# Attention tails in their units' rows, step 0's products between the attention units, and x's operands made by VectorE and ScalarE at the chunk ends

## What is computed

```
kv  = einsum('bhsd,bhse->bhde', k, v)             # 4 batches, 8 heads, 576 tokens, head size 64
out = einsum('bhsd,bhde->bhse', q, kv)
x   = out / sqrt(mean(out^2 over e) + 1e-6) * g_norm     # then [2304 tokens, 512]
h = x @ w_in1;  g = h * sigmoid(1.702 h);          x = g @ w_out1     # 512 -> 2048 -> 512
h = x @ w_in2;  g = max(h,0) + log1p(exp(-|h|));   out = g @ w_out2
```

## Time and profile before

| | |
|---|---|
| median of 3 runs | 854.32 us (853.38 to 855.62) |
| the profiled execution | 852.89 us, span 850.9 us |
| PE busy | 811.4 us, 95% of the span |
| DVE busy | 589.1 us, 69% |
| ACT busy | 417.4 us, 49% |
| POOL busy | 262.9 us, 31% |
| DMA | 139.26 MB, mean 164 GB/s |
| granted PE clock, 40 slices | 0.9 or more in all |

### The profile page before, as it was taken

How to read it: one execution, slowest core, us unless ns; L and a number is a source line. 1 busy time by engine, 2 the same in 40 slices (tenths; PEclk the granted TensorE clock), 3 DMA queues, 4 the chain that set the end, 5 groups by cost and what they waited for, 6 DMA issues and landing times.

```text
span 850.9 us, 12328 instructions
## 1 busy us (share of the span) xinstructions
PE 811.4 (95%) x4584; PEld 731.5 (86%) x4584; DVE 589.1 (69%) x1012; ACT 417.4 (49%) x800; POOL 262.9 (31%) x292
## 2 busy tenths in 40 slices
PE   6888999999999999999999998997999998999998
PEld 5788999988999988999987887886889887899896
DVE  3677567596656586666587777678776778776774
ACT  3663333233122133233257775665666665866765
POOL 4997787122124102345234423052100031000000
PEclk9999999999999999999999999999999999999999
DMA  9955646332843722854833544223252422262312
GB/s 309 339 211 177 239 152 267 154 112 87 284 173 122 275 87 88 301 221 155 309 126 112 212 168 166 86 96 122 104 186 87 172 89 87 97 237 87 108 67 74
DMA packets 25674, 139.26 MB, mean 164 GB/s; under 512 B 2448, under 2 KB 8208, under 8 KB 18448
## 3 DMA queue, kind: packets, MB, share of 16 engines
q1 hardware_dynamic: 25040, 138.16, 44.9%
q10 hardware_dynamic: 576, 0.33, 0.1%
HBM read 104.40 MB, written 34.08 MB: 163 GB/s over the span
## 4 chain that ended last, share of the span: by engine, by line
PE 74%; DVE 13%; ACT 5%; DMA 5%; issue 3%; ACTq 0%; DVEq 0%
PE ps L628 35%; PE ps L683 15%; PE ps L691 14%; PE ps L688 8%; DMA kv_in_sb<-k_v 4%; DVE gs_f L971 2%; DVE gs_f L1012 2%; DVE ex L1009 2%; DVE gs_f L1016 2%; DVE gs L1020 2%; DVE xs L946 2%; ACT gs L816 1%; ACT ex L792 1%; ACT fix L794 1%; ACT ex L790 1%
## 5 line engine op out<-in xcount | busy, mean ns | idle before, releaser
L628 PE MATMUL ps<-xs,w_in 128*128 128x384 f32 x2016 | 412.9, 340 | 23.6 <-DVE gs_f L971 16.5
L628 PEld LDWEIGHTS ps<-xs,w_in 128*128 128x128 f32 x2016 | 355.9, 188 | 56.6 <-issue 16.2
L683 PE MATMUL ps<-w_out,gs 128*128 128x512 f32 x864 | 228.0, 396 | 0.6 <-DVE gs L1020 0.4
L971 DVE TENSOR_TENSOR gs_f<-ps,gs_f 128x384 f32<-128x384 f32 x240 | 132.9, 555 | 137.2 <-PE ps L628 136.3
L683 PEld LDWEIGHTS ps<-w_out,gs 128*128 128x128 f32 x864 | 160.8, 189 | 25.8 <-issue 2.2
L691 PE MATMUL ps<-gs,w_out 128*128 128x512 f32 x576 | 148.2, 392 | 0.0
L691 PEld LDWEIGHTS ps<-gs,w_out 128*128 128x128 f32 x576 | 105.6, 188 | 16.4
L452 POOL TENSOR_TENSOR w_in<-w_in_f,w_in 128x256 fp32r<-128x256 f32 x112 | 93.5, 872 | 71.3 <-ACT w_in L821 71.0
L784 ACT ACTIVATE lg<-gs_f 128x384 f32<-128x384 f32 x72 | 37.8, 525 | 133.9 <-DVE gs_f L971 133.9
L816 ACT CAST gs<-gs_f 128x384 fp32r<-128x384 f32 x96 | 49.0, 510 | 94.0 <-DVE gs_f L1016 93.1
L1020 DVE TENSOR_TENSOR gs<-gs_f,gs 128x384 fp32r<-128x384 f32 x96 | 59.3, 617 | 41.3 <-ACT gs L816 38.2
(11 more groups left out here) (66 smaller groups left out, 571.1 us busy)
## 6 DMA issues: line engine op xcount, KB each, us to landing
w_in<-w_kept SPq DMA_DIRECT2D x40, 1792.0 KB, 7.4
w_kept<-w_in SPq DMA_DIRECT2D x16, 1792.0 KB, 10.4
kv_in_sb<-k_v SPq DMA_DIRECT2D x16, 512.0 KB, 10.8
w_in_f<-w_in SPq DMA_DIRECT2D x16, 512.0 KB, 4.1
w_out_f<-w_out SPq DMA_DIRECT2D x16, 512.0 KB, 8.1
q_sb<-q_t SPq DMA_DIRECT2D x16, 288.0 KB, 11.1
out<-xy SPq DMA_DIRECT2D x18, 256.0 KB, 7.8
tail_sb<-k_v SPq DMA_DIRECT2D x3, 256.0 KB, 12.5
```

The source lines that it names most:

```text
L628: mm = nc.tensor.matmul(ps[:, bank, 0:HALF], w[:, wp, W_OF[k], cols], xs[:, k, xp, t], start=(new and t == 0 and (wp, xp) == (HI, HI)), st ...
L683: mm = nc.tensor.matmul(ps[:, acc_bank(1, j), 0:DM], g[:, j * P:(j + 1) * P], w, start=new, stop=done)
L971: nc.vector.tensor_tensor(to, bank, other, ALU.add).then_inc(added, 1)
```

## The change

Four parts.

1. **k and v.** The host lays out k and v anew: per partition the four tiles of an even unit, then a tile whose rows 0 to 63 are its tail of k and the rest zero, a tile with both units' tails of v, then the odd unit's four tiles and a tile with its tail of k in rows 64 to 127. Each unit is one transfer (5120 or 4608 bytes a partition, before 4096 and the tails apart). `kv_in_sb` has 3 slots of two units, q 6 slots instead of 8. `tail_sb`, its memset and its four transfers are gone. ACT waits for the gain before its first `gain`, no longer before its second copy. The raw `w_in` of pair 2 and `w_out` of pair 0 are loaded after all units.
2. **Step 0.** P1 after unit 10, P2 (now second) after unit 12, P6 after unit 14; ACT copies C11 out of PSUM (`keep_c11`), so that the bank is free. U2 and U3 stand before unit 15's scaling. POOL makes x's slots before weight pair 2. DVE makes x's raw sums two by two behind units 9 and 10, before one by one behind units 9 to 12.
3. **Chunk ends.** POOL makes nothing of x. DVE makes the four sums of the late ends in the third and second step from the end (`ahead`) and all low parts, ACT all roundings. At the ends of layer 1 the same instructions stand in other places.
4. **`w_out` of layer 2** for pairs 6 and 7 is swapped in steps 26 and 28, not 24 and 25.

```
-    Q_SLOTS = 8
+    KV_SLOTS = 3
+    Q_SLOTS = 6
-        X_EARLY = (B11, B21, T2, T3, T4, T1, B22)
+        X_EARLY = (B11, B21, B22, T2, T3, T4, T1)
-        SWAP_FROM = PHASE1 - STEPS + 2
+        SWAP_AT = (18, 19, 20, 21, 22, 23, 26, 28)
 # SP
-                if u >= UNIT_SLOTS:
-                    sp.wait_ge(kv_done, u - UNIT_SLOTS + 1)
+                if u >= 2 * KV_SLOTS:
+                    sp.wait_ge(kv_done, (u // 2 - KV_SLOTS) * 2 + 2)
+                sp.dma_start(kv_in_sb[:, u // 2 % KV_SLOTS, kv_piece(u)], k_v[u // 2, :, kv_piece(u)]
+                             ).then_inc(kv_in[u % (2 * KV_SLOTS)], 16)
-            W_AT = {1: 0, 4: 1, 8: 2}
+            W_AT = {1: 0, 4: 1}
+            load_w_out(0, 0)
+            load_raw(2)
             keep(0)
 # PE, after unit u
-                if u == UNITS - 3:
+                if u == P1_UNIT:
                     product(0, P1)
+                if u == P2_UNIT:
+                    product(0, P2)
                 if u == UNITS - 2:
                     product(0, P6)
 # ACT, in a step; "late" is the end of steps 31 and 39
+                if ends_late:
+                    round_x(ci + 1, B11)
+                if begins_late:
+                    round_x(ci, T4)
+                    round_x(ci, T1)
                 if m > PHASE1:
                     round_g(m - 1, C12)
...
+                if ends_late:
+                    round_x(ci + 1, T2)
+                    round_x(ci + 1, B21)
+                if begins_late:
+                    round_x(ci, B22)
                 if m >= PHASE1:
                     round_g(m, C11)
...
+                if ends_late:
+                    round_x(ci + 1, T3)
                 hidden(m, C21)
 # DVE, in a step
+                ahead = X_LATE_FROM <= ci + 1 < 2 * CHUNKS and p in (STEPS - 3, STEPS - 2)
+                if begins and ci < X_LATE_FROM:
+                    low_x(ci, T3)
                 if m > 0:
                     add(m, U2)
                 if m > PHASE1:
                     low_g(m - 1, C12)
                 if begins:
                     low_x(ci, T4)
+                if ends or ends_late:
+                    low_x(ci + 1, B11)
+                if ahead:
+                    raw_x(ci + 1, T3 if p == STEPS - 3 else T4)
                 if phase:
                     add(m, U3)
                     softplus(m, C11)
...
+                if ends_late:
+                    low_x(ci + 1, T2)
+                if begins:
+                    low_x(ci, T1)
                 if phase:
                     low_g(m, C11)
                 add(m, C21_ADD)
...
+                if ends_late:
+                    low_x(ci + 1, B21)
                 if begins:
                     low_x(ci, B22)
+                if ahead:
+                    raw_x(ci + 1, T2 if p == STEPS - 3 else T1)
                 add(m, C22_ADD)
...
                 if ends:
-                    low_x(ci + 1, T3)
+                    low_x(ci + 1, B21)
+                    low_x(ci + 1, T2)
```

More of the change, by code:

```diff
@@ L57, in build @@
     UNITS, _, S = q_t.shape
+    KV_ROW = k_v.shape[2]
     T, DM = out.shape
@@ L188, in turn_bank, with kv_piece, kv_tile @@
             return TURN_ODD if u % 2 else TURN_EVEN
+        def kv_piece(u):
+            even = (2 * MAIN + 2) * P
+            return slice(even, KV_ROW) if u % 2 else slice(0, even)
+        def kv_tile(u, t):
+            slot = u // 2 % KV_SLOTS
+            first = kv_piece(u).start + 2 * t * P
+            k = kv_in_sb[:, slot, first:first + P]
+            if t == MAIN:
+                first = 2 * MAIN * P
+            return k, kv_in_sb[:, slot, first + P:first + 2 * P]
         def q_tokens(u, slot):
@@ L215, in g_high, with products_done @@
             return gs[:, m % 2, f, HI, half * HALF:(half + 1) * HALF]
+        P1_UNIT, P2_UNIT = 10, 12
+        def products_done(m, k):
+            place = {P2: P6, P6: P2}.get(k, k) if m == 0 else k
+            return PRODUCTS * m + place + 1
         def split_buffer(d):
@@ L600, in product @@
                         pe.wait_ge(x_split_early, X_EARLY.index(k) + 1)
-                    elif m // STEPS >= X_LATE_FROM and k in (B11, B21):
-                        pe.wait_ge(x_split_late, 2 * (2 * (m // STEPS - X_LATE_FROM) + (B11, B21).index(k) + 1))
                     else:
@@ L977, in _ @@
                     dve.wait_ge(x_made, 2 * PAIRS)
-                if 0 <= u - 2 * PAIRS - 1 < 4:
-                    raw_x(0, X_RAW_ORDER[u - 2 * PAIRS - 1])
-            add(0, U2)
+                    raw_x(0, T3)
+                    raw_x(0, T2)
+                if u == 2 * PAIRS + 2:
+                    raw_x(0, T4)
+                    raw_x(0, T1)
             def hidden_of(m, tile):
-                return ps[:, BANK_A, 0:HALF] if tile == C11 else hid(m, tile)
+                return ps[:, BANK_A, 0:HALF] if tile == C11 and m > 0 else hid(m, tile)
             def gate(m, tile):
@@ L1026, in _ @@
                 ends, begins = p == STEPS - 1 and m < ALL - 1, p == 0 and ci > 0
-                own_sums = ends and ci + 1 < X_LATE_FROM
+                ends_late = ends and ci + 1 >= X_LATE_FROM
+                ends = ends and not ends_late
+                ahead = X_LATE_FROM <= ci + 1 < 2 * CHUNKS and p in (STEPS - 3, STEPS - 2)
                 if m > PHASE1:
@@ L1040, in _ @@
                     softplus(m, C11)
-                elif m == 0:
-                    add(m, U3)
-                    gate_product(m, C11)
-                else:
+                elif m > 0:
                     gate_product(m, C11)
@@ L1065, in _ @@
                     low_x(ci, B22)
+                if ahead:
+                    raw_x(ci + 1, T2 if p == STEPS - 3 else T1)
+                add(m, C22_ADD)
+                if m == 0:
+                    gate_split(m, C11)
                 if phase:
```

202 lines of the change are left out of this document (84 added, 118 removed).

## The result

| | before | after |
|---|---|---|
| median of the runs | 854.41 us (853.38 to 855.62, 4 runs) | 830.03 us (828.63 to 830.67, 4 runs) |
| profiled execution | 852.89 us, span 850.9 | 830.67 us, span 828.9 |
| step 1's P1 starts at | 68.44 us | 62.98 us |

The ratio is 0.9712, with a 95% interval of 0.9694 to 0.973: the change is 2.9% faster. 830 us lies inside the range, 6 us above the forecast of 824.

What follows compares the result with a forecast made beforehand. PE's own pace was taken as the bound, with 31.0 us of waits around chunk ends and in steps 25 to 29, besides attention waits. Terms 7.0 + 5.9 + 17.6 = 30.5 us gave 824 us, range 816 to 836.

Steps and rivals of the forecast that it cites:

- Late ends: Steps 25 to 29, 31 to 33, 39 and 40: without POOL's work on x, 17.6 us saved; bounds 9 and 20.
- Ends of layer 1: Steps 7, 8, 15, 16, 23 and 24: reordered DVE work removes waits, 5.9 us saved; bounds 3 and 9.
- The new wait of P6 behind T2's low part: Ends of layer 1: P6 comes 1.1 us late in step 8, 0.4 in step 16, some 1.3 in step 24.
- Attention: Attention and step 0: step 1's P1 comes at 61.4 us and a C22 wait goes, 7.0 us saved; bounds 3 and 9.
- The start: I take 1.6 us: Start of the attention: the 1.74 us wait for tails goes, less a bigger kv of unit 0; 1.6 us saved.
- Rival 1: Attention: transfers keep holding it, at 300 GB/s step 1 starts at 65 us; 827.5 us, chance 0.13.
- Pair 2, moved last, is ready at 67 for step 2 at 77: Attention's end: POOL's work on weight pair 2, moved last, is ready at 67 us, ahead of step 2 at 77.
- Rival 2: Chunk ends: new waits take half the gain, 12 us instead of 23.5; 835.5 us, chance 0.13.
- Rivals 3 to 5: All waits go, 816.3 us, chance 0.08; slower through DVE's and ACT's queues, 867, 0.02; nothing that counts, 854, 0.01.

Runs made afterwards that it cites:

- b_late: Kernel before with only the two chunk ends inside layer 2 changed (POOL makes nothing of x there); 837.8 us, ratio 0.9814.
- a_swap: Changed kernel with `w_out` of pairs 6 and 7 of layer 2 swapped in steps 24 and 25 again; 831.08 us (1 run).
- a_best: Changed kernel with T2's low part and ACT's copies moved earlier, U2 ahead of C12's gate, pair 3's rounding later, sums of pairs 14 and 15 held; 822.48 us.
- a_t2: Changed kernel with T2's low part ahead of B21's at the ends of layer 1; 829.09 us (1 run).
- a_start: Changed kernel with unit 1's k and v asked for behind unit 0's q, not ahead of it; 829.88 us, ratio 0.9727.
- a_hold: Changed kernel where POOL waits for U2 of step 1 before it begins with weight pair 2; 834.88 us, ratio 0.9784.
- a_hold2: Kernel of a_hold with ACT's rounding of weight pair 3 moved behind the sigmoid of C12 in step 1; 833.32 us, ratio 0.975.
- a_u2: Changed kernel where DVE makes U2 of step 1 ahead of the gate of step 0's C12; 830.59 us, ratio 0.9717.

## Why the prediction was right, and where it wasn't

The gain of the span was 22.0 us of 30.5 forecast. Each of the three terms came out smaller than forecast and step 1 added a cost, so no miss hid another.

**Late ends.** Right in mechanism and size: 17.6 us forecast, 16.2 measured; for steps 28 to 41 alone 17.4 forecast and 17.2 measured, in the change and in b_late alike. POOL is idle from step 29 on, and DVE's L1023 (before L1016) takes at most 0.56 us from 517 us on. Two terms were off. ACT's copies of the sums (1.0 us at 33 and again at 41) weren't in the sum: I looked for places for the roundings and not at what else stood in ACT's list there. And 25 to 27 got 0.9 us worse, not 0.2 better: POOL's sums of pair 15 began 3.2 us ahead of step 27 before; now they wait 3.3 us for the raw load and begin as step 27 does, beside its softplus. With `w_out` in its old steps (a_swap) step 27 takes 16.19 us again. That the sums do their harm beside DVE there isn't shown: holding them until U2 of step 27 (a_best) won nothing, as ACT then waited for them.

**Ends of layer 1.** 5.9 forecast, 4.6 measured. The new wait of P6 behind T2's low part is there, 0.66 and 1.67 us instead of 1.1 and 1.3, the wait for T1 is gone, and a_t2 shows the cause. What was missing is 23's and 24's share: with `w_out` of step 24 away from POOL's list, the sums of pair 14 moved up to 429.76 us, onto the gates ahead of step 24 (with it back, in a_swap, step 23 takes 15.98 us and not 16.53).

**Attention.** 5.5 us at step 1's P1 instead of 7.0. "The start: I take 1.6 us" was the step that failed: the first k and v land at 5.58 us, not 4.5, so unit 0's products end 0.6 us earlier and not 1.6. Why is open but for 0.4 us, which a_start gives to unit 1's transfer beside them. Unit 9's sum comes at 36.24 (34.7 forecast), unit 15's raw output at 52.89 (52.0), and from there to step 1's P1 it takes 10.1 us (9.4). The rest went as walked: the P1 behind P3 waits 1.52 us (forecast 1.5), PE waits for nothing of POOL's, and from unit 9's to unit 13's sum it is 13.74 us (13.5 to 14.2). Rival 1 didn't come: the stream ran at 407 GB/s, PE waited 0.9 us for k and v behind the start. By this the 358 GB/s of the Trainium skill's "DMA: Bandwidth & Descriptors", section "Where 436 GB/s comes from", is no limit of this kernel's stream.

**Step 1** is where most of the miss lies, 4.4 us. The step that failed is "Pair 2, moved last, is ready at 67 for step 2 at 77": I priced POOL's moved work by its reader alone, and cost it at nothing. It was ready at 72.0 us, well in time. But the same collision with DVE that I took for the cause of 19 us in layer 2 works here too, on three gates in a row with U2 behind them; a_hold shows the gates at 1.5 us when POOL is silent, a_hold2 a step 1 of 15.80 us, and a_u2 and a_best that the loss came through two places, U2's in DVE's list and the rounding's in ACT's. The rule of the Trainium skill that the prediction names, "SBUF — State Buffer", section "Who interferes with whom", speaks of instructions like L999 and L1007, two of a gate's three; the prediction has it beside the attention's sums (1.9 us as a bound; one sum did take 2.27 us instead of 0.95) and not beside step 1's gates.

Rival 2, new waits that take half of what the ends give, was right in kind and too high in price: the ends keep 10.1 us of waits instead of 7.5, not 19. Rivals 3 to 5 didn't come.

## What to carry to other kernels

Work that is moved has three prices, and each is read at its own place: its reader, the engine that it runs beside, and what is queued behind every instruction that waits for it. Here POOL's pair 2 was in time for its reader and cost some 4 us through the second; held back, it made step 2's P1 7 us late through the third, in ACT's queue. When a wait is named after an engine that had long been done, follow the other operand: the 6.8 us "for POOL" were an add behind a gate, behind a sigmoid, behind a rounding.
